# Softmax's shift and sum folded into per-block exponentials, and the first operands of x made early by DVE and POOL

## The reference, cut to what matters

```python
# attention: batch 4, heads 8, seq 576, head_dim 64, window 64
scores = scale * np.matmul(q, k.transpose(0, 1, 3, 2))
mask = (rel >= 0) & (rel < window)
scores = np.where(mask, scores, -1000000000.0)
scores = scores - np.max(scores, axis=-1, keepdims=True)
attn = np.exp(scores)
attn = attn / (np.sum(attn, axis=-1, keepdims=True) + 1e-09)
attn_out = np.matmul(attn, v)
x = attn_out.transpose(0, 2, 1, 3).reshape(B * S, H * D)      # 2304 x 512
# mixture of 8 experts, F = 1024
logits = x @ w_gate; P = exp(logits - logits.max())
for _ in range(8): P /= P.sum(1) + 1e-9; P /= P.sum(0) + 1e-9; P *= N / E
for e in range(E): out += P[:, e:e+1] * (np.maximum(x @ w1[e], 0.0) @ w2[e])
```

## Time and profile before

| | |
|---|---|
| median of 3 runs | 1643.51 us (1642.75 to 1644.31) |
| profiled execution, its own time | 1639.98 us |
| its span in the trace | 1638.2 us |
| PE busy | 1608.7 us, 98% of the span |
| POOL, DVE, ACT busy | 995.9, 742.3, 526.1 us |
| chain that ended last | PE 95%, DVE 3%, POOL 1%, DMA 1% |

### The profile page before, as it was taken

One profiled execution on the slowest core, in us unless ns is written; L12 is line 12 of the kernel. 1 busy time (PEld: TensorE's weight loads), 2 busy tenths in 40 slices (PEclk: granted clock), 3 DMA queues, 4 the chain that ended last, 5 costly groups with the idle time before them and its releaser, 6 DMA issues.

```text
span 1638.2 us, 24414 instructions
## 1 busy us (share of the span) xinstructions
PE 1608.7 (98%) x8958; PEld 1443.1 (88%) x8958; DVE 742.3 (45%) x1263; ACT 526.1 (32%) x751; POOL 995.9 (61%) x644
## 2 busy tenths in 40 slices
PE   7988999999999999999999999999999999999999
PEld 6977888888888888888888888888888888888888
DVE  5766734434434344344344344344344344344343
ACT  3432323233232333332323323334333232332321
POOL 5945465565655778556556565687655655656552
PEclk9979999999999999999999999999999999999999
DMA  9822111212212113121121221213212112122111
GB/s 253 214 55 77 52 66 63 77 51 77 76 52 77 54 74 116 52 77 65 63 77 51 77 76 52 77 54 108 83 52 77 66 63 77 51 77 76 52 64 39
DMA packets 35437, 124.54 MB, mean 76 GB/s; under 512 B 4288, under 2 KB 4416, under 8 KB 35392
## 3 DMA queue, kind: packets, MB, share of 16 engines
q1 hardware_dynamic: 35392, 123.93, 22.7%
HBM read 119.19 MB, written 4.72 MB: 76 GB/s over the span
## 4 chain that ended last, share of the span: by engine, by line
PE 95%; DVE 3%; POOL 1%; DMA 1%; issue 0%; ACT 0%; DVEq 0%; POOLq 0%
PE ps L403 16%; PE ps L404 16%; PE ps L402 16%; PE ps L386 14%; PE ps L382 14%; PE ps L384 14%; PE ps L298 1%; PE ps L320 1%; PE ps L310 1%; PE ps L330 1%; DMA qk_buf<-qk 1%; DVE xv_lo L785 0%; DVE row_sum L907 0%; DVE p_t L764 0%; DVE prob L932 0%
## 5 line engine op out<-in xcount | busy, mean ns | idle before, releaser
L650 POOL TENSOR_TENSOR w_lo<-w_raw,w_hi 128x1792 fp32r<-128x1792 f32 (+1 forms) x101 | 391.8, 3879 | 531.2 <-ACT w_hi L494 530.3
L536 ACT ACTIVATE h_hi<-ps 128x384 fp32r<-128x384 f32 x384 | 189.4, 493 | 964.7 <-DVE ps L809 449.6
L402 PE MATMUL ps<-w_hi,h_hi 128*128 128x512 f32 x1152 | 454.0, 394 | 2.6 <-POOL w_lo L657 2.6
L403 PE MATMUL ps<-w_lo,h_hi 128*128 128x512 f32 x1152 | 456.1, 396 | 0.0
L404 PE MATMUL ps<-w_hi,h_lo 128*128 128x512 f32 x1152 | 455.9, 396 | 0.0
L386 PE MATMUL ps<-xv_hi,w_lo 128*128 128x384 f32 x1344 | 453.3, 337 | 0.0
L382 PE MATMUL ps<-xv_hi,w_hi 128*128 128x384 f32 x1344 | 451.4, 336 | 1.1 <-DVE h_lo L791 1.1
L384 PE MATMUL ps<-xv_lo,w_hi 128*128 128x384 f32 x1344 | 450.8, 335 | 0.0
L791 DVE SCALAR_TENSOR_TENSOR h_lo<-ps,h_hi 128x384 fp32r<-128x384 f32 x384 | 214.2, 558 | 366.0 <-ACT h_hi L536 365.2
L382 PEld LDWEIGHTS ps<-xv_hi,w_hi 128*128 128x128 f32 x1344 | 253.8, 189 | 30.8 <-DVE h_lo L791 1.5
L384 PEld LDWEIGHTS ps<-xv_lo,w_hi 128*128 128x128 f32 x1344 | 253.7, 189 | 29.1
(11 more groups left out here) (64 smaller groups left out, 964.9 us busy)
## 6 DMA issues: line engine op xcount, KB each, us to landing
w_raw<-w SPq DMA_DIRECT2D x192, 512.0 KB, 3.9
qk_buf<-qk SPq DMA_DIRECT2D x16, 576.0 KB, 7.7
v_win<-v SPq DMA_DIRECT2D x16, 288.0 KB, 4.5
out<-x_raw SPq DMA_DIRECT2D x18, 256.0 KB, 3.2
v_win<-v SPq DMA_DIRECT2D x16, 256.0 KB, 6.7
const_sb<-consts SPq DMA_DIRECT2D x1, 160.0 KB, 3.6
wg<-w_gate SPq DMA_DIRECT2D x1, 16.0 KB, 5.0
```

The costliest lines, as they stand in the source:

```text
L402: nc.tensor.matmul(ps_y[t], h_hi[slot][:, f, c], w2_hi[slot][:, f, :], start=opens, stop=False)
L403: nc.tensor.matmul(ps_y[t], h_hi[slot][:, f, c], w2_lo[slot][:, f, :], start=False, stop=False)
L536: nc.scalar.activation(h_hi[slot][:, f, half * HT:(half + 1) * HT], o, ACT.Relu)\
L650: last = nc.gpsimd.tensor_tensor(w1_lo[:, slot, c], w1_raw[:, slot, (lo + 1) * BLK:(hi + 1) * BLK], w1_hi[:, slot, c].bitcast(F32), ALU.su ...
```

## The change

Two things change, both ahead of step 1 of the experts.

Softmax: DVE makes `max_bias` = -scale x maximum (9 numbers a partition) behind the maximum; ACT takes the exponentials block by block, nine instructions of 64 columns a round, each with its own bias and with its sum as accumulator output; POOL's `shift` and DVE's sum fall away. In the built program each of these 144 exponentials is followed by an instruction of ACT that writes the accumulator out.

The first third's operands of x: high parts on DVE (`x_split`), in rounds 7, 8, 10, 11, 13, 14 and behind the last; differences and rests on POOL; the order in which the rests come is that of `X_TURN`. The `sums` of w1 for step 1 go from round 8 to behind the last rest, w1's split and rests for step 0 to rounds 4 to 6.

```diff
+X_TURN = [P1, P2, P5, P6, P7, P3, P4]
@@ PE, product
-                    pe.wait_ge(xv_lo_ready, s * PRODUCTS + k + 1)
+                    pe.wait_ge(xv_lo_ready, s * PRODUCTS + (k if s else X_TURN.index(k)) + 1)
@@ ACT
             def exp(p):
-                act.wait_ge(shifted, p + 1)
-                e = sc[:, p % SCR, :, :]
-                nc.scalar.activation(e, e, ACT.Exp, scale=float(D) ** -0.5).then_inc(exp_done, 1)
+                act.wait_ge(bias_ready, p + 1)
+                k = p % SCR
+                for i in range(QB):
+                    e = sc[:, k, i, :]
+                    last = nc.scalar.activation(e, e, ACT.Exp, bias=max_bias[:, k, i:i + 1], scale=SCALE,
+                                                accum_out=soft_sum[:, k, i:i + 1])
+                last.then_inc(exp_done, 1)
@@ POOL
-                    pool.wait_ge(x_taken, 2 * PAIRS)
+                    pool.wait_ge(x_taken, PAIRS + 2 if i == T1 else 2 * PAIRS)
...
             for p in range(NP):
-                shift(p)
                 if p:
                     weigh(p - 1)
...
+                if p == 8:
+                    x_rest(0, P1, 1)
+                if p == 9:
+                    x_rest(0, P2, 2)
                 if p == 10:
+                    x_sum(0, T1)
+                if p == 11:
+                    x_rest(0, P5, 3)
+                    x_sum(0, T2)
+                if p == 12:
+                    x_rest(0, P6, 4)
+                if p == 13:
+                    x_sum(0, T3)
+                if p == 14:
+                    x_rest(0, P7, 5)
+                if p == 15:
+                    x_sum(0, T4)
             weigh(NP - 1)
+            x_rest(0, P3, 6)
+            x_rest(0, P4, 7)
+            sums(1, 1, 16)
             w1_rest(1, 1)
@@ DVE
                 nc.vector.tensor_reduce(row_max[:, k, :], sc[:, k, :, :], AX_X, ALU.max).then_inc(max_done, 1)
+                dve.wait_ge(max_done, p + 1)
+                nc.vector.tensor_scalar(max_bias[:, k, :], row_max[:, k, :], -SCALE, None, ALU.mult)\
+                  .then_inc(bias_ready, 1)
...
-                nc.vector.tensor_reduce(soft_sum[:, k, :], sc[:, k, :, :], AX_X, ALU.add).then_inc(sum_done, 1)
...
+            def x_split(k):
+                if k in (P1, P2):
+                    dve.wait_ge(x_taken, PAIRS)
+                elif k == P3:
+                    dve.wait_ge(x_taken, 2 * PAIRS)
+                else:
+                    dve.wait_ge(t_done, {P5: 1, P6: 2, P7: 3, P4: 4}[k])
+                nc.vector.tensor_copy(xv_hi[:, x_slot(0, k), :, :], x_operand(0, k)).then_inc(xv_hi_ready, 1)
...
-                if p == 12:
-                    x_rest(P1)
...
+                if p in (7, 8):
+                    x_split((P1, P2)[p - 7])
+                if 10 <= p < 15 and p != 12:
+                    x_split({10: P5, 11: P6, 13: P7, 14: P3}[p])
             turned(NP - 3)
             soften(NP - 1)
-            x_rest(P4)
-            x_rest(P3)
+            x_split(P4)
             add_u2(0, 0)
```

More of the change, by code:

```diff
@@ L20 @@
 SINKHORN = 8
+SCALE = float(D) ** -0.5
 EPS = 1e-9
@@ L102, in build @@
             row_max = sb(att, "row_max", [P, SCR, QB])
+            max_bias = sb(att, "max_bias", [P, SCR, QB])
             soft_sum = sb(att, "soft_sum", [P, SCR, QB])
@@ L138, in build @@
         max_done = sem("max_done")
[L139 removed]
+        bias_ready = sem("bias_ready")
         exp_done = sem("exp_done")
[L141 removed]
         inv_done = sem("inv_done")
@@ L502, in x_split @@
             def x_split(s, k):
-                if k in (P1, P2, P3):
-                    if s == 0:
-                        act.wait_ge(x_taken, 2 * PAIRS)
-                else:
+                if k not in (P1, P2, P3):
                     act.wait_ge(t_done, s * 4 + {P5: 1, P6: 2, P7: 3, P4: 4}[k])
-                if s and k >= XRING - PRODUCTS:
+                if k >= XRING - PRODUCTS:
                     act.wait_ge(prod_done, PRODUCTS * (s * PER_SB - 1) + (k - (XRING - PRODUCTS)) + 1)
@@ L587, in _ @@
                     x_copy(p - 3)
-                if p == 6:
+                if p == 4:
                     w1_split(0, 0, 0)
-                if p == 11:
-                    x_split(0, P1)
-                if p == 13:
-                    x_split(0, P6)
-                    x_split(0, P2)
-                if p == 14:
-                    x_split(0, P7)
-                    x_split(0, P5)
-                if p == 15:
-                    x_split(0, P4)
-                    x_split(0, P3)
             exp(NP - 1)
@@ L673, in x_sum, with x_rest @@
                 nc.gpsimd.tensor_tensor(t_raw[:, i, :, :], a, b, ALU.subtract).then_inc(t_done, 1)
-            def x_rest(s, k):
-                pool.wait_ge(xv_hi_ready, s * PRODUCTS + k + 1)
+            def x_rest(s, k, nth=0):
+                pool.wait_ge(xv_hi_ready, s * PRODUCTS + (nth or k + 1))
                 at = x_slot(s, k)
@@ L679, in x_rest @@
                                         ALU.subtract).then_inc(xv_lo_ready, 1)
-            def shift(p):
-                pool.wait_ge(max_done, p + 1)
-                e = sc[:, p % SCR, :, :]
-                nc.gpsimd.tensor_tensor(e, e, row_max[:, p % SCR, :].unsqueeze(2).to_broadcast([P, QB, WINDOW]),
-                                        ALU.subtract).then_inc(shifted, 1)
             def weigh(p):
@@ L699, in _ @@
             for p in range(NP):
-                shift(p)
                 if p:
                     weigh(p - 1)
-                if p == 5:
+                if p == 3:
                     sums(0, 0, 16)
-                if 6 <= p < 11:
-                    w1_rest(0, 0, p - 6, p - 5)
+                if 4 <= p < 7:
+                    w1_rest(0, 0, (0, 2, 4)[p - 4], (2, 4, 7)[p - 4])
                 if p == 8:
-                    sums(1, 1, 16)
+                    x_rest(0, P1, 1)
+                if p == 9:
+                    x_rest(0, P2, 2)
                 if p == 10:
-                    w1_rest(0, 0, 5, 7)
-                if 11 <= p < 15:
-                    x_sum(0, p - 11)
+                    x_sum(0, T1)
[10 more added lines that the diff above has]
+                    x_sum(0, T4)
             weigh(NP - 1)
+            x_rest(0, P3, 6)
+            x_rest(0, P4, 7)
+            sums(1, 1, 16)
             w1_rest(1, 1)
@@ L777, in soften @@
                 dve.wait_ge(exp_done, p + 1)
-                nc.vector.tensor_reduce(soft_sum[:, k, :], sc[:, k, :, :], AX_X, ALU.add).then_inc(sum_done, 1)
-                dve.wait_ge(sum_done, p + 1)
                 nc.vector.reciprocal(soft_inv[:, k, :], soft_sum[:, k, :]).then_inc(inv_done, 1)
-            def x_rest(k):
-                dve.wait_ge(xv_hi_ready, k + 1)
-                at = x_slot(0, k)
-                nc.vector.tensor_tensor(xv_lo[:, at, :, :], x_operand(0, k), xv_hi[:, at, :, :].bitcast(F32),
-                                        ALU.subtract).then_inc(xv_lo_ready, 1)
+            def x_split(k):
[6 more added lines that the diff above has]
+                nc.vector.tensor_copy(xv_hi[:, x_slot(0, k), :, :], x_operand(0, k)).then_inc(xv_hi_ready, 1)
             def rest(n, slot, o, f, half, i):
@@ L946, in _ @@
                     soften(p - 1)
-                if p == 12:
-                    x_rest(P1)
-                if p == 14:
-                    x_rest(P6)
-                    x_rest(P2)
-                if p == 15:
-                    x_rest(P7)
-                    x_rest(P5)
+                if p in (7, 8):
+                    x_split((P1, P2)[p - 7])
+                if 10 <= p < 15 and p != 12:
+                    x_split({10: P5, 11: P6, 13: P7, 14: P3}[p])
             turned(NP - 3)
             soften(NP - 1)
-            x_rest(P4)
-            x_rest(P3)
+            x_split(P4)
             add_u2(0, 0)
```

2 lines of the change are left out of this document (removed).

## The result

| | before | after |
|---|---|---|
| median of 4 runs | 1643.34 us (1642.75 to 1644.31) | 1655.87 us (1654.55 to 1657.56) |
| first profiled execution, its own time | 1639.98 us | 1655.92 us |
| its span | 1638.2 us | 1654.1 us |
| a second profiled execution | 1643.78 us | 1657.57 us |
| PE, DVE, ACT, POOL busy | 1608.7, 742.3, 526.1, 995.9 us | 1615.7, 725.2, 557.2, 987.1 us |

The change makes the kernel slower: ratio 1.0069 [1.0057, 1.0081], 12.5 us between the medians. The forecast was 1664.0 (1651 to 1678): the direction and the mechanism held, its 20.5 us were too many. First the stages, as windows with the columns of the earlier trace rows; the first two answer to its two rows, the last is a stretch behind the second product.

The account below looks back on a forecast made before the run. PE bounds the kernel, so delay in the first 125 us is paid in full. P1 15.6 late, tail 2.3 and slow clock 2.6 make 20.5 us; on profiled 1639.98 that is 1660.5, plus 3.5 gives 1664.0 (1651 to 1678).

Parts of the forecast that it names:

- c: ACT's time for one 64-column exponential with its readout: 0.38 us (0.17 to 0.53), built from 0.17 + 0.21.
- the ring: Softmax's loop own, merge, maximum, bias, nine exponentials: a round cannot be shorter than 2.57 + 9c = 5.99 us, before 4.23.
- own(10): ACT's own of round 10 starts at 68.7 instead of 56.71, 12.0 us late, after ten rounds of 5.99.
- The waits for POOL's differences: DVE's x_split in rounds 10, 11, 13 waits behind weigh: 1.7, 3.4, 1.7 us over the ring.
- the clock: Half clock on PE after those gaps, for mixes and transposes on the ring: 1.5 us (0 to 4) before own(15).
- What comes back: From own(15) to P1, without DVE's x_rest: 7.2 us instead of 14.6, so 7.4 regained.
- The tail: P1 to mix(15) takes 12.6 us, 2.3 more, through weigh(15), last copy, rests, sums, w1_split and x_copy(14).
- The clock term behind mix(15): From mix(15) to the second product, products and gate tiles at half clock: 2.6 us more (0 to 4).
- The lock in the ring: Rival: each round's bias on DVE meets a POOL instruction, up to 2 us a round: +42, 1686; chance 0.02.
- The cheap exponential: Rival: c about 0.22, readout nearly free, ring 4.55 hidden under PE's gate rounds: +10, 1654; chance 0.16.
- Faster: Rival: waits for POOL hidden, c 0.17, P1 7.2 us behind own(15), tail costs 2.3: -5, 1638; chance 0.05.
- the 3.5 us: Added to the profile-based 1660.5 because the median of the runs is 3.5 above the profile, giving 1664.0.

Follow-up runs that it names:

- no_readout: Changed kernel without the exponentials' accumulator output, DVE summing as before; pointer bias and nine blocks stay: ratio to before 1.0058, +10.1 us.
- splits_late: Changed kernel with DVE's copies of T1 to T3 one round behind their differences, rests moved to match, P3's copy in round 13: ratio to before 1.0012, +2.4 us.
- planned: Changed kernel reordered: one POOL operation of x a round, differences a round or more ahead of copies, w1 sums in round 7: ratio to before 0.9978, -4.2 us.
- x_only: Changed kernel with the softmax of before (POOL's shift, one exponential of 576 columns, DVE's sum): ratio to before 1.0043, +7.2 us.
- softmax_only: Kernel before with only the new softmax, x operands made as before: ratio to before 1.0020, +3.6 us.
- own first: Changed kernel with own(p) moved ahead of exp(p-1) on ACT: ratio to before 1.0063, +10.8 us.

## Why the prediction was right, and where it was too high

By its own steps, against the first profiles:

| step | forecast | measured |
|---|---|---|
| a block's exponential with readout, c | 0.38 us | 0.333 |
| the ring | 2.57 + 9c = 5.99 | 2.51 + 3.00 = 5.50 |
| own(10) | 68.7 | 64.41 |
| bias to bias in rounds 10, 11, 13 | 7.7, 9.4, 7.7 | 7.63, 9.41, 7.63 |
| own(10) to own(15) | 38.3 | 38.50 |
| own(15) to P1 | 7.2 | 6.97 |
| P1 to mix(15) | 12.6 | 13.04 |
| mix(15) to second product | 18.3 | 16.17 |
| second product, against 124.66 | +20.5 | +14.4 |

**The ring was right, its price too high.** Everything of it that was read from rows held (2.57 against 2.51). The price c was built from two parts, and both were wrong in ways that partly cancelled. The exponential alone comes every 0.24 us and not every 0.17: `no_readout` shows it, with a record of 338 ns where the forecast built 0.26. The readout costs 0.09 and not 0.21, because most of its 189 ns lie beside the neighbours. The difference of 0.047 us, 9 blocks in 10 rounds, is 4.2 us, the size of the miss at own(10) (4.3). Two smaller misses cancel beside it: 2.57 against 2.51 is 0.6 us in ten rounds, and w1_split in round 4 cost 1.2 us instead of 0.5 (own(4) to own(5) is 6.74 instead of 5.50). The kernel did sit above the limit of 0.31 from which even PE's gate rounds lose, but by little: PE idled 0.1 to 0.2 us a gate round by the ring's measure (5.50 against 5.33), not 0.7.

The forecast set a rule beside this: a bias through a per-partition pointer adds about 93 ns (the Trainium skill, ScalarE: Activation LUTs, What ACT_TABLE_LOAD costs). The runs bear it out in size, 338 - 263 = 75 ns more in the record and 0.07 in the spacing. No run here has the same exponential without the pointer, so the 0.07 stand on a built number. So leaving the rule out made c too low by about 0.07, and giving the readout the fixed part of a whole instruction made it too high by 0.12; the second mistake was the larger. That c came out as near as 0.047 is partly luck, and with the rule alone put right it would have been further off (0.47).

**The waits for POOL's differences were right to 0.1 us**, in their places, order and length, and the experiments make them the largest term (9 to 10 us with the copies that `splits_late` moved). A chain that is read row by row, with what stands behind the waiting instruction, can be summed. Against the ring as it was, 5.50, they come to 2.1 + 3.9 + 2.1 = 8.1 us; own(10) to own(15) lost 38.50 - 27.5 = 11.0. The other 2.9 are what is left over the ring in the two rounds without such a wait: from bias(12) to bias(13) 5.80 us (83.75 to 89.55), from bias(14) to bias(15) 8.03 (97.18 to 105.21). ACT's timeline of these rounds, with PE's rows of round 14:

```profile
83.66 0.70 ACT L531 COPY x_raw<-ps 128x384 f32<-128x384 f32 x2 [3.46 <-PE ps L323]
84.25 0.36 ACT L518 ACTIVATE sc<-sc,max_bias 128x64 f32<-128x64 f32 x1
...
95.80 2.19 PE L323 MATMUL ps<-p_t,v_win 128*64 128x64 f32 x36 [2.71 <-DVE p_t L764]
97.92 2.18 PE L313 MATMUL ps<-const_sb,probs 128*128 128x128 f32 x9
98.61 0.36 ACT L518 ACTIVATE sc<-sc,max_bias 128x64 f32<-128x64 f32 x1
100.03 2.83 PE L301 MATMUL ps<-qk_buf 64*64 64x64 f32 x36
...
102.91 0.64 ACT L525 COPY sc<-ps 128x576 f32<-128x576 f32 x1 [1.21 <-PE ps L301]
```

In round 14 PE comes out of a gap of 2.71 us at half clock. Mix, transposes and scores take 2.19, 2.18 and 2.83 us instead of 1.27, 1.20 and 2.08, and own(15) waits for the scores: 2.5 us, which the forecast put at 1.5 (0 to 4). One path I did not name: x_copy(p-3) stands between own(p) and exp(p) on ACT and waits for PE's mix. In round 12 it makes the exponentials 0.3 us late (bias done at 83.92, first exponential at 84.25), and that is the 0.3 there. In rounds 11 and 14 it makes them 1.26 us late (74.51 to 75.77, 97.35 to 98.61), but the copy of T2 and PE's scores end later still, so it costs nothing. That the total came to 38.3 against 38.50 is partly luck: the ring was taken 0.5 us too long in each of these two rounds, and the clock and x_copy 1.3 us too short.

**What comes back was right** (7.2 against 6.97), and with it the reason, since `splits_late`, `planned` and `x_only` have the same 6 to 7 us there and `softmax_only`, which keeps DVE's rests, has 12.2.

**The tail was right up to mix(15), and its cause only half.** In the changed kernel the chain is the one forecast: weigh(15), two rests, four sums, the split, x_copy(14), mix(15). But without the sums mix(15) gains only 1.1 of the 2.7 us, since another path stands just under this one: transposes and products behind mix(14), partly at half clock (0.77, 1.6 us). The last copy met weigh(15) and took 2.46 us instead of the 0.6 that I gave it. That cost little: mix(14) follows P1 by 4.35 us as in the kernel before, and P3's rest on POOL took 2.13 us instead of 1.81. `planned`, which has neither the sums in the tail nor a low clock behind mix(14), is back at 10.3. The clock term behind mix(15), 2.6 us (0 to 4), was wrong: 16.17 against 15.74 is 0.4.

**The rivals.** The lock in the ring was rightly priced at nothing in this kernel: the new bias took 0.17 us on average. The lock was elsewhere, in the last copy, at a price of about 0.3 us. The cheap exponential (c 0.22) was out: the ring did bound the gate rounds. "Faster" failed where the forecast said, at a difference behind a weigh that needs the reciprocal.

**The sum.** The misses are 4.3 at own(10), 2.1 behind mix(15), and 0.4 the other way between them (0.2 - 0.2 + 0.4): 20.5 - 6.0 = 14.5 against 14.4 measured. From that to the medians' 12.5 there is one more step, the profile that it was set on. The forecast added 3.5 us to a profile that lay below its kernel's median; the changed kernel's first profile lay on its median, and has 1.5 us more behind the second product: 8.1 = 6.0 + 3.5 - 1.5, to rounding. So the 3.5 us were a term that did not carry over. The second profile of before has the second product 3.7 us later than the first, and 2.7 of that are PE's waits for the DMA of v, which neither profile of the changed kernel shows. The 1.5 us behind the second product, which the forecast put at nothing, are the longer low clock there (0.66 instead of 0.83).

What stays open besides: how the 12.5 us divide exactly. The two halves add up to 10.8, within the intervals' reach of 12.5. The softmax half costs 3.6 us alone, 5.3 beside the waits (12.5 - 7.2, `x_only` against the changed kernel) and 3.8 in the planned order (8.0 - 4.2); these do not differ beyond the intervals. Breaking the ring inside the changed kernel gave only 1.7, which is not the price of the ring, since own first makes the reciprocal late as well.

## What to carry to other kernels

Splitting one instruction into nine to fold a pass into it moves work from an engine that had time to one that closes a ring; find the ring first, and compare its length with the bound engine's round. Where a consumer's producer depends on the same round's result, the consumer waited here for the whole way (4 to 6 us), whatever room the engines had: put the consumer one round later. Judge the two halves of a change apart: here another order of the same x operations with the old softmax is 8.0 us faster than before, where the change as made is 12.5 us slower.
